# A head's fifteen maximum blocks laid 3, 2, 1, 2, 3 + 1, 2, 1 over its nine steps instead of 2, 2, 2, 2, 2 + 1, 2, 2

## What is computed

```python
q_pool = q.reshape(B, H, S // 2, 2, D).mean(axis=3)          # B 4, H 8, S 1152, D 64: 576 pooled queries
scores = scale * np.matmul(q_pool, k.transpose(0, 1, 3, 2))  # 576 x 1152 for each head
scores = scores - np.max(scores, axis=-1, keepdims=True)
attn = np.exp(scores)
attn = attn / (np.sum(attn, axis=-1, keepdims=True) + 1e-09)
out = np.matmul(attn, v)
```

## Time and profile before

| | before |
|---|---|
| median of 3 runs | 1131.06 us (1129.37 to 1131.52) |
| the profiled execution | 1127.29 us |
| its span, from the first to the last instruction | 1125.5 us |
| TensorE matmul busy | 1092.2 us, 97% of the span |
| VectorE busy | 741.0 us, 66% |
| ScalarE busy | 531.8 us, 47% |
| GpSimd busy | 459.0 us, 41% |
| mean granted TensorE clock | 0.992 of full speed |

### The profile page before, as it was taken

The page is one execution under the profiler, slowest core; times in us unless marked ns, Lnnn a source line. Parts: engine busy times, 40 slices in busy tenths (PEclk is TensorE's granted clock), DMA queues, the critical chain, the costliest instruction groups (busy, mean ns, idle before and its releaser), DMA issues.

```text
span 1125.5 us, 22186 instructions
## 1 busy us (share of the span) xinstructions
PE 1092.2 (97%) x7849; PEld 921.4 (82%) x7849; DVE 741.0 (66%) x1706; ACT 531.8 (47%) x945; POOL 459.0 (41%) x337
## 2 busy tenths in 40 slices
PE   7999999999999999999799999999899999999996
PEld 5777777777777777777598999999799999999995
DVE  7767767887778877786446777777465655566641
ACT  3566655655555665554225444444054344254320
POOL 0768877777876788777600000000000101111100
PEclk9999999999999999999899999999899999999999
DMA  5273225223322233311659014447385281231100
GB/s 132 66 232 75 64 75 149 72 70 95 104 65 74 75 86 96 81 37 33 231 177 354 28 38 179 165 182 277 127 336 175 75 328 37 78 138 40 44 10 15
DMA packets 74398, 132.61 MB, mean 118 GB/s; under 512 B 11040, under 2 KB 29472, under 8 KB 74320
## 3 DMA queue, kind: packets, MB, share of 16 engines
q1 hardware_dynamic: 43568, 50.84, 16.9%
q10 hardware_dynamic: 26096, 68.96, 16.7%
q0 software_dynamic: 4656, 11.79, 3.0%
HBM read 106.12 MB, written 19.24 MB: 111 GB/s over the span
## 4 chain that ended last, share of the span: by engine, by line
PE 94%; DVE 2%; issue 1%; ACTq 1%; ACT 0%; SPq 0%; DMA 0%; POOL 0%; DVEq 0%; POOLq 0%
PE PS L765 24%; PE PS L600 14%; PE PS L514 11%; PE PS L566 9%; PE PS L573 8%; PE PS L583 7%; PE PS L778 6%; PE PS L782 6%; PE PS L779 6%; PE PS L615 1%; PE PS L638 1%; PE PS L797 1%; DVE mx L1070 1%; ACTq L846 0%; DMA moe<-xs 0%
## 5 line engine op out<-in xcount | busy, mean ns | idle before, releaser
L454 POOL TENSOR_TENSOR arena_a<-arena_a,arena_p 128x576 f32<-128x576 f32 x222 | 330.3, 1488 | 85.3 <-ACT arena_p L883 62.7
L1070 DVE TENSOR_REDUCE mx<-PS 128x1 f32<-128x384 f32 (+1 forms) x480 | 246.3, 551 | 108.9 <-PE PS L566 105.3
L765 PE MATMUL PS<-moe,W 128*128 128x128 f32 x2432 | 279.0, 276 | 1.5 <-ACT moe L969 1.5
L765 PEld LDWEIGHTS PS<-moe,W 128*128 128x128 f32 x2432 | 276.2, 192 | 3.7 <-ACT moe L969 1.9
L883 ACT ACTIVATE arena_p<-PS 128x576 f32<-128x576 f32 x288 | 187.6, 653 | 132.0 <-PE PS L583 131.5
L573 PE MATMUL PS<-QHT,KA 128*128 128x288 f32 x576 | 182.0, 329 | 0.0
L1175 DVE TENSOR_TENSOR W2L<-W2R,W2H 128x1024 fp32r<-128x1024 f32 x144 | 169.8, 1220 | 16.4 <-ACT W2H L855 15.9
L566 PE MATMUL PS<-KA,QHT 128*128 128x384 f32 (+1 forms) x480 | 173.7, 364 | 2.2 <-DVE mx L1070 2.0
L583 PE MATMUL PS<-QLT,KB 65*128 65x288 f32 x576 | 171.1, 301 | 0.2 <-ACT QLT L894 0.2
L855 ACT CAST W2H<-W2R 128x1024 fp32r<-128x1024 f32 x148 | 144.3, 1048 | 50.4 <-PE PS L782 41.6
L600 PE MATMUL PS<-arena_p,arena_a 128*64 128x288 f32 x1152 | 160.5, 414 | 0.0
(11 more groups left out here) (181 smaller groups left out, 1154.1 us busy)
## 6 DMA issues: line engine op xcount, KB each, us to landing
W<-in_moe_w ACTq DMA_DIRECT2D x16, 2048.0 KB, 14.9
W2R<-in_moe_w ACTq DMA_DIRECT2D x16, 2048.0 KB, 9.8
moe<-xs SPq DMA_DIRECT2D x40, 258.0 KB, 2.7
arena_a<-in_k SPq DMA_DIRECT2D x32, 288.0 KB, 3.0
arena_a<-in_v SPq DMA_DIRECT2D x32, 288.0 KB, 2.8
KB<-KA SPq DMA_DIRECT2D x32, 288.0 KB, 3.1
arena_a<-in_q SPq DMA_DIRECT2D x32, 256.0 KB, 3.2
xs<-padrow SPq DMA_DIRECT2D x9, 258.0 KB, 3.6
```

Source lines behind the costliest of these rows:

```text
L454: nc.gpsimd.tensor_tensor(Acc[u], Acc[u], P[u][:, t, :], ALU.add).then_inc(acc_step, 1)
L765: last = nc.tensor.matmul(PS[:, HB + f // 4, (f % 4) * PN:(f % 4 + 1) * PN], W1[s][:, d, f * PN:(f + 1) * PN], xT[:, d, :], start=(d == 0) ...
L1070: vec.reduce_max(mx3[0:n, t, c:c + 1], PS[0:n, MXB + b % 2, 0:KB_], AX.X).then_inc(pr_max, 1)
```

## The change

TensorE issues the same fifteen blocks for a head, each with the same wait, at other places among the nine steps. Steps 0 to 6 held 2, 2, 2, 2, 2 and one behind the third V group, 2, 2. They now hold 3, 2, 1, 2, 3 and one behind the third V group, 2, 1. The third block of step 0 stands between the K transposes and the first V group, the third of step 4 directly behind the second and ahead of the third V group. On VectorE the first two `k_low` now follow b2 instead of b1, and the routing steps of place 9 follow b10 instead of b9.

```diff
@@ TensorE, body(h) @@
-                    if after and t < 7:
+                    if after and t < 6 and t != 2:
                         prior(h + 1, next(blocks))
...
                             trans_k(h + 2, 0)
                             if h == FIRST:
                                 keep_busy(14)
+                        if after:
+                            prior(h + 1, next(blocks))
                         if before:
                             weighted(h - 1, 0)
...
                     if t == 4:
+                        if after:
+                            prior(h + 1, next(blocks))
                         if before:
                             weighted(h - 1, 2)
                             sums(h - 1)
@@ VectorE, body(h) @@
-                        if b == 1:
+                        if b == 2:
                             k_low(h + 2, 0)
                             k_low(h + 2, 1)
...
-                    route_in(b)
+                    route_in({5: 5, 10: 9}.get(b))
```

## The result

The changed kernel takes 1159.01 us (median of 6 runs) against 1131.88 us for the kernel before (6 runs alongside). One run of each six was in a much slower state (2000.99 and 1791.8 us); the ratio is that of the other five, 1.0232 with a 95% interval of 1.0209 to 1.0256, which is 26 us (24 to 29), while the medians of all six are 27.1 us apart. The forecast was 1155 us within 1148 to 1160; the median of the five is 1157.74. The profiled execution took 1156.83 us, its span is 1155.1; against the 1127.29 and 1125.5 of before that is 29.5 us more.

What follows compares the result with a forecast made beforehand. TensorE, busy 97% of the span, was taken as the bound. 29 heads at 0.83 (24.1 us), the last head 1.1 and the filling bodies -1.1 gave +24 on 1131.1, so 1155 us; range 1148 to 1160, 8 in 10.

Steps and rivals of the forecast that it cites:

- The price of a close block: On TensorE, block b + 2 can start without waiting only 1.09 us after b's start: 0.38 + 0.55 + 0.16.
- 0.68 forecast: At step 4, b10 directly behind b9 waits 0.68 us for its bank, ahead of the third V group.
- the 0.09 and 0.15: Waits in a changed head: b5 behind the small K transpose 0.09 us, b13 taking over b12's wait 0.15 us.
- 0.17: At step 0, b2 behind the four transposes waits 0.17 us for the maximum of b0.
- +0.83 a head: Waits in each of heads 1 to 29 sum to 1.09 us against 0.26 before, 0.83 us more.
- Strict order on VectorE: VectorE cannot take the maximum of b8 ahead of `q_low`; 0.2 of b10's 0.68 us comes from this.
- The walk: One middle head followed instruction by instruction on TensorE and VectorE; its 0.83 us was applied to 29 heads, 24.1 us.
- The filling bodies: In h = -1 and 0, maxima b3 to b5 end earlier, 0.5 to 0.6 us each, say -1.1 us.
- The low price: Rival: a late block loses only 0.05 us beyond the maximum; +0.63 a head, 18 us, 1149 us; chance 15%.
- Hiding half the stall: Rival: half of b10's stall (0.34 us) falls into existing waits; about 0.4 a head, +12 us, 1143; chance 5%.
- The faster case: Rival: b10 finds its bank free and waits of b4 and b5 are saved; 4.4 us less, 1127; chance 3%.
- The clock rival: Rival: new waits lower TensorE's clock in each fourth head; 24 us more, 1179; chance 3%.

Runs made afterwards that it cites:

- Numbers 1 and 2: 1: changed kernel without the extra block ahead of the third V group, ratio 1.0036; 2: changed kernel with the old first half, ratio 1.0180.
- numbers 5 and 6: 5: kernel before with b4, b5 and b12 moved apart, ratio 0.9929; 6: kernel before with only b12 moved, between the two transposes back, ratio 0.9965.
- Number 3: Changed kernel with `q_low` on VectorE moved from behind b7 to behind the maximum of b10; 1153.81 us, ratio 1.0198 to the kernel before.
- The first half alone: Changed kernel keeping the extra block ahead of the first V group, without the one ahead of the third; 1136.18 us, ratio 1.0036 to the kernel before.
- number 7: The first half alone, with the old first-half order in the three bodies that follow the ranks of a batch; 1137.0 us in one execution.

## Why the prediction was right, and which terms were off

- **The price of a close block.** 1.09 us from the start of b - 2 to that of b held wherever it was tried. b10 waited 0.69 for 0.68 forecast, b5 and b13 the 0.09 and 0.15, and b2's wait is 0.17: in the changed head the four transposes start at 419.80, so b2 is ready at 420.24, and its matmul ends at 420.30 + 0.45, as if it had begun at 420.41. The sum, +0.83 a head, was measured as 17.23 against 16.41. Numbers 1 and 2 split it into 0.14 and 0.67, numbers 5 and 6 turn its sign.
- **Strict order on VectorE.** The forecast gave 0.2 of the 0.68 to `q_low`. Number 3 found 0.22. This is what the Trainium skill says in "TensorE: Matmul & The Clock Gate" (Architectural detail) of the other engines' queues, and the trace agrees: with `q_low` out of the way the maximum of b8 comes that much earlier, and while it stood there nothing passed it.
- **Heads after a batch: missed.** The walk took the maximum of b0 at 400.70 as the same in all heads. In three it is late, and the delay that b2's place at step 1 had mostly hidden is paid: 0.78 us each on top of the 0.83. The head behind each gives 0.10 back, which leaves 2.0 us.
- **The filling bodies: too much.** The forecast gave them -1.1 us. The first V group comes at 39.36 against 39.58, and it now has b2 (0.18 and 0.17 of wait) ahead of it, so by my estimate they gave back about 0.57. With b2 ahead of `k_low` it is b5 that waits. Its weight load in the two bodies:

```profile
15.05 0.19 PEld L566 LDWEIGHTS PS<-KA,QHT 128*128 128x128 f32 x1 [1.21 <-DVE mx L1074]
...
28.24 0.19 PEld L566 LDWEIGHTS PS<-KA,QHT 128*128 128x128 f32 x1 [0.98 <-DVE mx L1074]
```

  The wait of the earlier trace rows moved from b4 to b5 and did not go.
- **The sum.** From the first to the last V group the changed kernel takes 26.7 us more: 22 plain heads at 0.83 (18.2), three after a batch at 1.61 (4.8), the three that follow them at 0.73 (2.2) and 1.5 for the last two. Less 0.2 at the start, the attention is 26.5 us longer where +24 was forecast for it, and the ratio's 26 (24 to 29) agrees. Both misses went the same way, 2.0 and 0.5, so they did not cancel; the median of all six runs lies 1 us inside the range's upper end.
- **The rivals.** The low price (1149, 0.63 a head) fell with the 0.83. Hiding half the stall (1143) fell with b10's 0.69, which reached the V group in full. The faster case would need b10's bank free; it was 0.69 late. The clock rival fell too: over 530 us of the attention, with a wait of 0.68 in each head, the clock stayed at full speed. The stretch in the changed kernel (us, busy by engine, PEclk, DMA share, GB/s):

```profile
30.00:560.00 530.00, 515.06 (x3651) 386.07 (x3650) 411.44 (x861) 294.28 (x585) 384.44 (x263) 1.00 0.30 81
```

  The Trainium skill warns in the same page (A second HAM failure mode) of a clock that falls from short idles while cycling through PSUM banks. It did not happen here at 97% busy (515.06 of 530).

What stays open: behind the last V group the twelve profiles of all kernels here took 582.1 to 586.0 us, and the two of the kernel before are the shortest, so about 1 us there may or may not belong to the change. The first half alone cost 4.1 us by its ratio and 6.0 between its first and last V group. The start differs by 3 us between its two profiles, and in the one that starts later `q_low` of h = 0 had begun just behind a GpSimd addition and taken 1.70 us (at 33.44) instead of 0.48 (at 31.56); that this is all of the 3 us is not shown.

## What to carry to other kernels

Two buffers between a producer and a consumer are a matter of distances, not of averages: VectorE idled over 100 us waiting for blocks, and yet laying three blocks close together cost 0.68 us a head. Work out for each item the distance to the one two before (start, production, consumption, handover) and give every item that much other work in between; here number 5 made the kernel 0.7% faster without taking any work away. Do the walk for every kind of iteration, since a delay that another order had hidden shows up only in the iterations that have it.

## What the runs showed of the hardware

- A VectorE addition or subtraction with both inputs in SBUF is stretched when it begins while a GpSimd addition is already running: `q_low` from 0.48 to 1.63 us (mean of 32: 483 and 1559 ns) by its place alone, the pooled queries from 0.47 to 1.70, while maxima that read PSUM stay at 0.55. Where the VectorE operation begins 0.05 or 0.06 us ahead, it keeps its 0.48 and the GpSimd addition takes 1.69 or 1.70 instead of 1.41. In the heads of number 7 a start 0.17 us later against the addition thus cost 1.2 us on VectorE. The Trainium skill names such contention in "GPSIMD Engine Reference" (1. Specifications: shared SBUF interfaces, with two SBUF inputs among the cases); the trace agrees.
- A matmul that waits for a bank starts effectively 0.15 to 0.16 us behind the releasing operation's end (0.10 with 64 columns of weights); its weight load, 0.19 us long (0.13), waits too, as its row shows.
- Breaking a group of V matmuls for one score block costs 0.34 us beside the block.
- At the attention's end TensorE idles and its clock falls. The waits that the profile names for it there are for VectorE (2.7 us) and ScalarE (2.0 and 0.7), and 3.6 us for nothing that it shows; none names a DMA. The same kernel had a mean of 0.80 over 34 us in one execution and 0.84 over 32 us in another, from these two rows (first and second profile of the changed kernel):

```profile
568.00:602.00 34.00, 24.89 (x198) 21.51 (x197) 13.46 (x58) 3.83 (x9) 13.18 (x13) 0.80 0.71 248
```

```profile
568.00:600.00 32.00, 24.42 (x203) 21.22 (x203) 13.45 (x58) 4.14 (x9) 13.15 (x13) 0.84 0.75 263
```

  In the first of them TensorE was busy for 1.65 of 4 us, then for 0.77 of 4, while the granted clock was 0.66 and 0.50, half of full speed (1.2 GHz):

```profile
576.00:580.00 4.00, 1.65 (x11) 1.51 (x11) 1.34 (x5) 0.32 (x1) 0.80 (x1) 0.66 1.04 408
580.00:584.00 4.00, 0.77 (x7) 0.64 (x7) 3.54 (x19) 0.49 (x2) 0.00 (x0) 0.50 1.00 411
```
